# A retention, soft-MoE and top-2-MoE kernel: last maximum joined by GpSimd, slots folded on TensorE, logit rows summed by VectorE, shorter chunk loads, another order of the SW block

## The reference

```python
for t in range(S):                       # q, k, v: (4, 8, 768, 64)
    state = gamma * state + einsum('bhd,bhe->bhde', k[:, :, t], v[:, :, t])
    y[:, :, t] = scale * einsum('bhd,bhde->bhe', q[:, :, t], state)
x = y as (3072, 512)                     # first MoE: soft, 8 experts, 4 slots each
logits = x @ phi                         # (3072, 32)
d = exp(logits - logits.max(0)); d /= d.sum(0) + 1e-9
slot_in = d.T @ x                        # over ALL tokens
slot_out[e] = relu(slot_in[e] @ w1[e]) @ w2[e]
c = softmax(logits, axis=1);  x = c @ slot_out
# second MoE: noisy top 2 of 8 experts, 512 -> 1024 -> 512
noisy = x @ w_gate + log1p(exp(x @ w_noise)) * noise
out = sum over the two best experts of weight * (relu(x @ w1[e]) @ w2[e])
```

## Time and profile before

| | us |
|---|---|
| median of 3 runs | 538.63 (537.22 to 539.7) |
| profiled execution, its own time | 540.1 |
| its span, first to last instruction | 538.3 |
| PE busy in the span | 496.1 (92%) |
| DVE / ACT / POOL busy | 274.6 / 185.5 / 255.3 |
| DMA engines, mean busy share 0 to 220 us | near 1.0, in single stretches less |
| chain that ended last | PE 83%, DMA 9%, issue 2%, DVE 2% |

### The profile page before, as it was taken

The page is one execution under the profiler, slowest core; times in us unless marked ns, Lnnn a source line. Parts: engine busy times, 40 slices in busy tenths (PEclk is TensorE's granted clock), DMA queues, the critical chain, the costliest instruction groups (busy, mean ns, idle before and its releaser), DMA issues.

```text
span 538.3 us, 13565 instructions
## 1 busy us (share of the span) xinstructions
PE 496.1 (92%) x4844; PEld 294.9 (55%) x4845; DVE 274.6 (51%) x443; ACT 185.5 (34%) x346; POOL 255.3 (47%) x217
## 2 busy tenths in 40 slices
PE   4998999997987568999999999999999999999995
PEld 3877787873577234444544544545545445445452
DVE  2674767575230796564646455464545332433422
ACT  0221222221003636846445363554442222223210
POOL 1221222212000013475777878786878766666553
PEclk9998999998997888999999999999999999999998
DMA  8999999998999999444465342132232332423410
GB/s 274 393 338 408 367 377 409 396 382 300 387 424 427 384 413 392 161 133 141 168 215 196 97 145 49 24 60 46 42 61 42 53 48 43 59 40 42 60 21 2
DMA packets 35096, 107.93 MB, mean 201 GB/s; under 512 B 11871, under 2 KB 13135, under 8 KB 32624
## 3 DMA queue, kind: packets, MB, share of 16 engines
q1 hardware_dynamic: 20880, 92.90, 44.8%
q0 software_dynamic: 14176, 14.49, 14.3%
HBM read 93.87 MB, written 29.43 MB: 229 GB/s over the span
## 4 chain that ended last, share of the span: by engine, by line
PE 83%; DMA 9%; issue 2%; DVE 2%; ACT 1%; SPq 1%; POOL 1%; DVEq 0%; POOLq 0%
PE ps L1022 51%; PE ps L1005 5%; PE ps L675 4%; PE ps L739 4%; DMA w_region<-moe_w 4%; DMA late_w1a<-chunks 3%; PE ps L888 3%; PE ps L859 3%; DMA w_region<-chunks 2%; PE ps L931 2%; PE ps L715 2%; PE ps L729 2%; PE ps L750 1%; PE ps L689 1%; PE ps L771 1%
## 5 line engine op out<-in xcount | busy, mean ns | idle before, releaser
L1022 PE MATMUL ps<-w_region,s_region 128*128 (+1 forms) x1304 | 290.3, 379 | 0.3 <-issue 0.3
L1022 PEld LDWEIGHTS ps<-w_region,s_region 128*128 128x128 f16 x1304 | 125.4, 98 | 141.5 <-issue 0.4
L1676 DVE SCALAR_TENSOR_TENSOR s_region<-ps,s_region 128x1024 f16<-128x1024 f32 x55 | 67.3, 1224 | 141.3 <-ACT s_region L1235 141.2
L1235 ACT ACTIVATE s_region<-ps 128x1024 f16<-128x1024 f32 x55 | 56.3, 1024 | 178.7 <-PE ps L1005 174.3
L625 POOL DMA_INDIRECT out<-s_region,rec_region x42 | 67.9, 1617 | 18.6 <-issue 11.6
L619 POOL DMA_INDIRECT out<-s_region,rec_region x41 | 54.9, 1339 | 37.2 <-DVE s_region L1706 32.6
L613 POOL DMA_INDIRECT rec_region<-records,idx x55 | 59.9, 1090 | 22.9 <-issue 16.4
L559 POOL TENSOR_TENSOR s_region<-w_region,s_region 128x512 f32<-128x512 f32 x14 | 14.6, 1043 | 51.7 <-PE ps L750 37.0
L1005 PEld LDWEIGHTS ps<-s_region,sw_region 128*128 (+1 forms) x440 | 29.6, 98 | 14.4 <-issue 1.2
L1706 DVE TENSOR_SCALAR s_region<-ps,rec_region,y_scale 128x512 f32<-128x512 f32 x42 | 33.8, 804 | 5.8 <-PE ps L1022 4.1
L1005 PE MATMUL ps<-s_region,sw_region 128*128 128x128 f16 x440 | 34.6, 219 | 0.6 <-ACT s_region L1230 0.4
(11 more groups left out here) (249 smaller groups left out, 576.0 us busy)
## 6 DMA issues: line engine op xcount, KB each, us to landing
w_region<-moe_w SPq DMA_DIRECT2D x49, 512.0 KB, 11.2
w_region<-moe_w SPq DMA_DIRECT2D x10, 2048.0 KB, 9.7
w_region<-chunks SPq DMA_DIRECT2D x26, 512.0 KB, 7.0
s_region<-moe_w SPq DMA_DIRECT2D x4, 2048.0 KB, 13.0
sw_region<-chunks SPq DMA_DIRECT2D x12, 512.0 KB, 7.2
late_w1a<-chunks SPq DMA_DIRECT2D x8, 512.0 KB, 7.6
w_region<-moe_w SPq DMA_DIRECT2D x3, 1024.0 KB, 8.3
s_region<-moe_w SPq DMA_DIRECT2D x5, 512.0 KB, 8.3
```

The lines of the kernel that those rows point to most:

```text
L1022: last = nc.tensor.matmul(bank[6 + r], h[:, r, f, :], w2b_parts[:, bass.ds(o, 1), part, f, :].rearrange("p e m -> p (e m)"), start=(first ...
L1235: nc.scalar.activation(h_hi[:, r, :, :].rearrange("p c t -> p (c t)").rearrange("p (a n) -> p a n", a=2), ps[:, 2 + 2 * r:4 + 2 * r, :], A ...
L1676: nc.vector.scalar_tensor_tensor(out=h_lo[:, r, :, :].rearrange("p c t -> p (c t)").rearrange("p (a n) -> p a n", a=2), in0=ps[:, 2 + 2 * ...
```

## The change

Five edits. (1) `load_qk` leaves out k by token for the last chunk of a sequence: 4 x 256 KB. (2) `logit_rows` transposes the 4 x 32 parts (128 x 128) into PSUM, and VectorE, ahead of its `keep_x_t` of two chunks later, sums the four parts and keeps the rows; ScalarE's copy is gone. `rows_at` and `turned_at` are now the same place. (3) For the last group, VectorE joins the partition maximum with the spread maximum of the groups before, and GpSimd's `partition_all_reduce` (128 x 32) gives the maximum to all partitions; `shift_last` reads it. `turn_max` and `join_max` remain, for `fade` alone, which ScalarE now takes after the exponential. GpSimd runs one such reduction on ones ahead of it, and VectorE zeroes `in_blocks`. (4) The slots are turned by four products with the stack (128 x 32 each) that accumulate the four parts, and VectorE writes the blocks straight from PSUM. (5) SW groups 0 to 3, 4 to 5, 6 to 7, with other banks and another order on TensorE, ScalarE and VectorE.

```diff
+                n = DM if g % NC == NC - 1 else 2 * DM
+                load_words(qk_in[g % QK_DEPTH][:, 0:n], g, 2 * DM, qk_full[g % QK_DEPTH])
...
-            pool.wait_ge(x_turned, NT)
-            nc.gpsimd.memset(in_blocks, 0.0).then_inc(blocks_zeroed, 1)
+            nc.gpsimd.partition_all_reduce(first_reduced, ones[:, 0:SL], P, MAX)
+            pool.wait_ge(group_max_ready, 1)
+            nc.gpsimd.partition_all_reduce(last_max, col_max[:, 0, :], P, MAX).then_inc(last_max_ready, 1)
...
-                nc.tensor.matmul(rows_at, logit_parts[t % 2], stack, start=True, stop=True).then_inc(logits_done, 1)
+                nc.tensor.transpose(rows_at, logit_parts[t % 2], ident[:, :]).then_inc(logits_done, 1)
...
-            spread_max(NG - 1)
...
-                last = nc.tensor.transpose(bank[4][:, d * P:(d + 1) * P], slot_acc[:, d * P:(d + 1) * P], ident[:, :])
+                last = nc.tensor.matmul(bank[4][:, d * SL:(d + 1) * SL], slot_acc[:, d * P:(d + 1) * P], stack,
+                                        start=(d == 0), stop=(d == DC - 1), skip_group_check=True)
...
# VectorE
+            def keep_logits(t):
+                dve.wait_ge(logits_done, t + 1)
+                nc.vector.tensor_reduce(logits[:, t, :], rows_at.rearrange("p (j s) -> p s j", j=REP), AX_X,
+                                        ALU.add).then_inc(logits_kept, 1)
+                if g == NG - 1:
+                    nc.vector.tensor_tensor(col_max[:, 0, :], col_max[:, 0, :], spread_at, ALU.max).then_inc(group_max_ready, 1)
+            def shift_last():
+                dve.wait_ge(last_max_ready, 1)
+                nc.vector.tensor_tensor(exp_last, logits[:, GROUPS[-1][0]:GROUPS[-1][1], :],
+                                        last_max.unsqueeze(1).to_broadcast([P, REP, SL]),
+                                        ALU.subtract).then_inc(cols_shifted, 1)
+            link(nc.vector.memset(in_blocks, 0.0))
+            keep_logits(NT - 2)
+            keep_logits(NT - 1)
             find_max(NG - 1)
+            shift_last()
             join_max(NG - 1)
-            shift_cols(NG - 1)
...
# TensorE, SW block
-            pe.wait_ge(*sw_kept(3))
-            turn_c(0, 0, 7)
+            pe.wait_ge(*sw_kept(4))
+            turn_c(0, 0, 6)
+            sw_spread_parts(4)
             hidden_b(0, 0, 0)
-            turn_c(1, 1, 7)
+            sw_spread_parts(5)
+            turn_c(1, 1, 6)
             sw_product(7)
-            for e in range(4, 7):
-                sw_spread_parts(e)
             first_rows(0, range(FC))
-            sw_spread_parts(7)
-            first_rows(1, range(FC))
+            first_rows(1, range(FC - 2))
+            sw_spread_parts(6)
+            sw_spread_parts(7)
+            first_rows(1, range(FC - 2, FC))
...
# ScalarE, SW block, whole order after sw_high of 0 to 3
-   keep 0, 1; sums 5; keep 2..7; sums 6; stage_c 0; keep_ct 0; stage_c 1; h_high 0; keep_ct 1;
-   high 4, 5, 6; sums 7; keep 8, 10, 12; high 7; keep 14; stage_c 2
+   sums 5; keep 0..3; high 4, 5; keep 4, 5; stage_c 0; keep 6; sums 6; keep_ct 0; keep 7, 8; h_high 0;
+   stage_c 1; keep 10; keep_ct 1; sums 7; high 6, 7; keep 12, 14; stage_c 2
# VectorE, SW block
-   w2b_low 0 (both halves); scales 1; low 4, 5, 6; keep 9, 11; scales 2; keep 13; low 7; keep 15; h_low 0
+   scales 1; low 4, 5; w2b_low 0 (half 0); keep 9; w2b_low 0 (half 1); keep 11; h_low 0; scales 2; low 6, 7; keep 13, 15
```

More of the change, by code:

```diff
@@ L215, in build_program @@
         rec_src_f = rec_src_flat.bitcast(F32).rearrange("p (k t w) -> p k t w", k=2, t=NT)
+        last_max = rec_region[:, 1700:1700 + SL].bitcast(F32)
+        first_reduced = rec_region[:, 1740:1740 + SL].bitcast(F32)
         rec_pad = sb("rec_pad", [1, RW], I32)
@@ L300, in build_program @@
         max_spread = sem("max_spread")
+        group_max_ready = sem("group_max_ready")
+        last_max_ready = sem("last_max_ready")
         cols_shifted = sem("cols_shifted")
@@ L377, in build_program @@
         FINE = 3
-        sw_out = [ps[:, 2 + e // 2, e % 2 * QF:(e % 2 + 1) * QF] for e in range(E - 1)] + [ps[:, 0, 0:QF]]
+        sw_out = [ps[:, 2 + e // 2, e % 2 * QF:(e % 2 + 1) * QF] for e in range(E)]
         SC = ((0, 1), (2, 3))
@@ L921, in sw_product @@
                 w = w1b_home[e].rearrange("p (c f) -> p c f", c=DC)
-                if e % 2 == 1 and e < E - 1:
+                if e % 2 == 1:
                     pe.wait_ge(sw_sum_ready, e)
-                if e == E - 1:
-                    pe.wait_ge(*sw_kept(6))
                 pe.wait_ge(w1b_full[e], 16 if e < FINE else 16 * REP)
@@ L1128, in _ @@
                         keep_den(g)
-            keep_logits(NT - 1)
             exp_slots(NG - 1)
@@ L1215, in _ @@
                 sw_high(e)
-            sw_keep(0)
-            sw_keep(1)
             sw_sums(5)
-            for unit in range(2, E):
+            for unit in range(4):
                 sw_keep(unit)
@@ L1229, in keep_ct @@
                 act.wait_ge(ct_turned, i + 1)
-                nc.scalar.activation(ct[:, r, :], bank[7 if isinstance(i, int) and i < 2 else r][:, 0:P // 2].bitcast(F16),
+                nc.scalar.activation(ct[:, r, :], bank[6 if isinstance(i, int) and i < 2 else r][:, 0:P // 2].bitcast(F16),
                                      ACT.Copy).then_inc(ct_ready, 1)
@@ L1236, in h_high @@
                                      ps[:, 2 + 2 * r:4 + 2 * r, :], ACT.Relu).then_inc(h_hi_ready, 1)
+            act.wait_ge(sw_scale_ready, 2)
+            for e in range(4, 6):
+                sw_high(e)
+            sw_keep(4)
+            sw_keep(5)
+            stage_c(0, 0, rec_arrival(0))
+            sw_keep(6)
             sw_sums(6)
-            stage_c(0, 0, rec_arrival(0))
             keep_ct(0, 0)
+            sw_keep(7)
+            sw_keep(8)
+            h_high(0, 0)
             stage_c(1, 1, rec_arrival(1))
-            h_high(0, 0)
+            sw_keep(10)
             keep_ct(1, 1)
-            act.wait_ge(sw_scale_ready, 2)
-            for e in range(4, 7):
+            sw_sums(7)
+            act.wait_ge(sw_scale_ready, 3)
+            for e in range(6, E):
                 sw_high(e)
-            sw_sums(7)
-            sw_keep(8)
-            sw_keep(10)
             sw_keep(12)
-            act.wait_ge(sw_scale_ready, 3)
-            sw_high(7)
             sw_keep(14)
@@ L1336, in join_max @@
                 link(nc.vector.tensor_reduce(found[:, g:g + 1], turned_at, AX_X, ALU.max))
+                if g == NG - 1:
+                    nc.vector.tensor_tensor(max_all[:, g:g + 1], max_new[:, g:g + 1], max_all[:, g - 1:g],
+                                            ALU.max).then_inc(max_diag_ready, 1)
+                    return
                 if g > 0:
@@ L1378, in sequence_copies @@
                     t = b * NC + c
+                    if t > 1:
+                        keep_logits(t - 2)
                     for g in group_ending(t - 1):
@@ L1603, in sw_low @@
             def sw_low(e):
-                dve.wait_ge(sw_hi_ready, e // 2 * 2 + 2 if e < 6 else e + 1)
+                dve.wait_ge(sw_hi_ready, e // 2 * 2 + 2)
                 nc.vector.scalar_tensor_tensor(out=sw_lo[:, e, :], in0=sw_out[e],
@@ L1671, in _ @@
                                     ALU.logical_shift_right).then_inc(tile_code_ready, 1)
-            w2b_low(0)
             def h_low(i, r):
@@ L1682, in _ @@
             sw_scales(1)
-            for e in range(4, 7):
+            for e in range(4, 6):
                 sw_low(e)
+            w2b_low(0, (0,))
             sw_keep(9)
+            w2b_low(0, (1,))
             sw_keep(11)
+            h_low(0, 0)
             sw_scales(2)
+            for e in range(6, E):
+                sw_low(e)
             sw_keep(13)
-            sw_low(7)
             sw_keep(15)
-            h_low(0, 0)
             for o in range(EARLY):
```

40 lines of the change are left out of this document (14 added, 26 removed).

## The result

Over 22 runs each the changed kernel took 536.82 us (535.48 to 539.28) and the one before 539.07 us (536.1 to 541.1): ratio 0.9966, 95% interval 0.9951 to 0.9982, so 1.8 us less (1.0 to 2.6); the ratio is taken over the single runs, and the two medians alone lie 2.25 us apart. The forecast was 2.0 less and inside 0.5%; the range of 533.6 to 539.5 holds the median. The profiled execution took 538.5 us with a span of 536.5 (before 540.1 and 538.3). In a later series of 12 runs, in which the kernel before had a median of 536.63 us, the same kernel's ratio was 0.9993 (0.9969 to 1.0017), 0.4 us less, an interval that holds no change; weighed by their intervals, the two series give an estimate of 0.9974, 1.4 us.

A forecast was written before the change was run, and what follows sets the result against it. The prediction took TensorE's loop, whose start hangs on the saturated DMA queue, to bound the kernel. Its terms, 1.1 + 0 + 0.66 + 0.28 + 0 = 2.0 us earlier, gave a median of 536.6 us, range 533.6 to 539.5.

The forecast's parts named there:

- What bounds it: TensorE's L1022 loop keeps its length; the time moves by exactly as much as the loop's start, which stands behind DMA.
- Part 1, 1.1 us: Attention: shorter chunk loads cut TensorE's waits for chunks, gain 1.1 us, bounds 0 to about 2.1.
- The wait at chunk 17 (0.50): Attention, at 85.14 us: the third shortened load lands early enough to cover TensorE's wait, gain 0.50 us.
- the 0.65: Attention, wait at 42.38 us: the queue is full, so later loads land 0.65 us earlier after the first shortened chunk.
- Part 2, 0: Attention's logit rows: transpose costs TensorE nothing, VectorE's sums fall into its wait; price 0, bounds 0 to +0.4 us.
- Part 3, 0.66: Join's last maximum: GpSimd's 32-column reduction taken at 1.1 us, last slot sums start 0.66 us earlier.
- part 4, 0.28: Join's slot folding: four products and a PSUM copy take 1.42 instead of 1.70 us; gain 0.28, bounds 0 to 0.7.
- The DMA stream follows w1a's start: Loads ahead of the loop: w1a starts 2.0 us earlier, so w1b's 201.69 becomes about 199.6.
- rival 1: Clock at the 42 us waits and w1a: shorter waits keep TensorE warm, 0.9 to 2.5 us more, 534.5; chance 0.17.
- Part 5, 0: SW block: product 7 comes 1.0 us later, its shorter chain wins 1.0; price 0, bounds -1.0 and +0.7.
- the prediction's own signs: Trace marks from attention to loop; wrong if expert 5's product to the loop (24.2 us) changes by over 0.7.
- The total of 2.0: Whole kernel: the five parts' sum, 2.0 us earlier, median 536.6, inside the 0.5% a measurement can tell.

The follow-up runs named there:

- the last two: Changed kernel, earlier register load, ScalarE's second w2b sums behind stage_c(3); the second also with VectorE's h_low(1) and keep_y(0) ahead of the scale: 1.0078 and 1.0016.
- p5_sw: The kernel before with part 5 alone (SW order, groups, banks): 1.0009 (0.9987 to 1.0031).
- p2_rows: The kernel before with part 2 alone (logit rows transposed, VectorE sums and keeps them, ScalarE's copy gone): 0.9997 (0.9974 to 1.0021).
- no_trial: The changed kernel without GpSimd's reduction of ones ahead of the last maximum: 0.9966 (0.9944 to 0.9988).
- join_only: The kernel before with parts 3 and 4 alone, also without the zeroing of in_blocks: 0.9979 (0.9957 to 1.0001).
- after_again: The changed kernel once more, unchanged, for a second profile: 0.9993 (0.9969 to 1.0017).
- wide_trial: The changed kernel with the trial reduction on 128 columns instead of 32: a single execution, 535.41 us.

## Why the prediction was right, step by step

- **What bounds it.** Held: the loop's length stayed at 312.4 to 313.0 us in every kernel but the last two, and the time of a profiled execution followed the loop's start.
- **Part 1, 1.1 us.** Half of it, by the traces. The wait at chunk 17 (0.50) is in one of nine kernels with the part, and there it is 0.34 (in the changed kernel's own profile it is not gone, as I had said it would be); the waits at 38 and 43 us, 1.31 and 1.26 there, remain, so the 0.65 is not seen. In the time nothing is shown: part 1 alone measured 0.9993 with an interval that holds both.
- **Part 2, 0.** Mis-sized: 0.04 us a chunk, about 0.8 us of TensorE. I had bounded it at 0.05 a chunk, which is 1.2 us, and then taken the middle; the sum of 128 columns on VectorE (0.29) was hidden, as worked out.
- **Part 3, 0.66, and part 4, 0.28.** 0.81 and 0.24, together 1.05 instead of 0.94. The reduction's row for four columns misled me (its 1.12 us read as a wait, see the end), the one for one column (0.40) was the right one; TensorE's own work capped the gain, so that an error of 0.67 us in the reduction moved the sum by 0.1 alone.
- **The DMA stream follows w1a's start.** Not shown: w1a starts 2.51 us earlier in the pair (131.00 against 128.49) and expert 5's product 3.4, but the stream's own length varies by 2.4 us between kernels with the same code up to there (53.1 to 57.3 over all), and of the part that came from the clock (rival 1) about 0.5 passed through it in the means.
- **Part 5, 0.** The working failed, the size of its effect was small. I let the later product 7 take back the 1.0 us that the shorter chain behind it wins. The chain won its 1.0 at full clock (11.8 to 10.75), but in p5_sw, where little stands in its way, product 7 started 0.3 us later than before and not 1.0: it is 1.0 later behind product 6, and product 6 is earlier. In the other profiles weights (0.46 to 0.58 us in four of the eight with the new order, in none with the old) and half clock over product 6 move it by more than the edit does (P7 12.7 to 14.9 in the new order, 12.4 to 14.6 in the old). By the tails less the 0.3 the part should bring 0 to 0.7 us, and the means of P7 and tail together differ by 0.35; alone it measured 1.0009 (0.9987 to 1.0031), which leaves room for 0.7 of gain at most, and the changed kernel without it 0.9983 against 0.9966. I had also not seen the register load, which bares TensorE for 1.2 us and led to half clock in two of five profiles, 0.7 us. What the part is worth in the time wasn't settled.

By the prediction's own signs the step from expert 5's product to the loop fails: it was to stay within 0.7 us of 24.2 and took 25.61 in the pair's profile (198.32 to 223.93). That expert's product came at 198.32, 1.3 us ahead of the 199.6 forecast, and the stretch behind it took 1.4 us more than forecast. The two cancel, and the loop starts at 223.93 where 223.9 was forecast. That is luck, since both swing by more than that with no edit behind it.

The total of 2.0 was met in the pair (1.8, interval 1.0 to 2.6) and not shown in the later series (0.4, -0.9 to 1.7). What the traces carry is 1.05 from parts 3 and 4, some 0.5 from part 1 and up to 0.8 from part 2, which was unforeseen and stands in the place of part 1's other 0.65. The pair's agreement is therefore no proof of each term, and in part luck.

## What to carry to other kernels

Where a term repeats by 0.02 us in every profile (a join, a chunk's period), measure it by landmarks of the trace; where a stage hangs on a saturated DMA queue, its length swung here by microseconds, and neither one profile nor a dozen runs told an edit of 1 us. Many small per-iteration differences deserve their product with the count before they are called zero. And a wait moved off one engine's order (ScalarE's 4 us of sums) must be followed through every queue that uses its result: here it came back as waits of 3.8 and 1.3 us in the loop.

## What the runs showed of the hardware

- `partition_all_reduce` (GpSimd, maximum, f32): 0.43 to 0.46 us for 32 columns, 0.72 for 128, 0.31 to 0.41 for one to three (0.61 once, in p2_rows, beside a long VectorE operation): a fixed cost and some 2.8 ns a column. The Trainium skill (GPSIMD Engine Reference, section 3.2 Cross-partition) gives 247,699 ns for a `tensor_reduce` along the partitions of 128 x 2048, by estimate 121 ns a column; that is another instruction, and the measurement of this one decides: 40 times less.
- The first such reduction of a program started 9.0 to 10.2 us behind GpSimd's work before it in the eight kernels with the trial, with no wait on anything (112.65 to 122.76 in the changed kernel). The traces have two MODIFY_POOL_CONFIG records at the start of this gap (112.84 and 112.87 there). In no_trial they stand at 111.95 and 111.99, 0.2 us behind the work before and ahead of the wait for the maximum, and the real reduction, 11.0 us behind that work, ran 0.14 us after its release; in the kernel before they stand at 130.5, and the reduction at 174.99. So the delay passes ahead of the semaphore wait. What fills it wasn't measured. With the trial GpSimd was ready for the real reduction only 0.29 to 1.49 us before the maximum came, so a shorter way there would have run into it.
- The 1.12 us for four columns that misled me reads as a wait for VectorE. The same call took 0.45 to 1.74 us in the fourteen profiles, and in every one it ended 0.16 to 0.27 us behind the end of one of VectorE's long f16 operations (128x2640). In join_only 187.80 + 1.53 = 189.33 against 187.85 + 1.74 = 189.59:

```profile
187.80 1.53 DVE L1649 TENSOR_TENSOR r_region<-s_region,count 128x2640 f16<-128x2640 f16 x1
187.85 1.74 POOL L608 PARTITION_ALL_REDUCE sw_sum<-sw_sum  x1 [1.14 <-ACT s_region L1180]
```

  In the join VectorE runs no such operation beside it. This is a reading of fourteen profiles; no run took the f16 operation away.
- TensorE at half clock in the tail: eight 512-column products took 3.29 and 3.40 us (changed kernel, p5_sw) instead of 1.89, behind a pause of 1.4 us. The stretch of the changed kernel, columns as in the earlier trace rows:

```profile
221.30:222.30 1.00, 1.00 (x4) 0.30 (x3) 0.29 (x2) 1.00 (x4) 0.50 (x2) 0.50 0.00 0
```

  The same pause left the clock full in three other profiles (after_again, no_trial, wide_trial).
